# Splitting the MLP weights into fp16 halves: half of the scalings moved from ScalarE to GpSimd, and each subtraction in one instruction

## The reference

```python
scores = scale * np.matmul(q, k.transpose(0, 1, 3, 2))
kth = np.partition(scores, -top_k, axis=-1)[..., -top_k:-top_k + 1]
scores = np.where(scores >= kth, scores, -1000000000.0)
attn = softmax(scores);  x = attn @ v          # 2304 rows of 512
h = x @ w_in                                   # 512 x 2048
x = (np.maximum(h, 0.0) + alpha * np.minimum(h, 0.0)) @ w_out
```

## Time and profile before

| | us |
|---|---|
| median of 3 runs | 1148.4 |
| lowest and highest | 1143.76 and 1156.6 |
| the profiled execution, its own time | 1143.76 |
| its span, first to last instruction | 1142.0 |
| busy in the span: PE, DVE, ACT, POOL | 929.2, 913.3, 624.2, 430.4 |

### The profile page before, as it was taken

The page is one execution under the profiler, slowest core; times in us unless marked ns, Lnnn a source line. Parts: engine busy times, 40 slices in busy tenths (PEclk is TensorE's granted clock), DMA queues, the critical chain, the costliest instruction groups (busy, mean ns, idle before and its releaser), DMA issues.

```text
span 1142.0 us, 22616 instructions
## 1 busy us (share of the span) xinstructions
PE 929.2 (81%) x6288; PEld 621.1 (54%) x6289; DVE 913.3 (80%) x2061; ACT 624.2 (55%) x1291; POOL 430.4 (38%) x597
## 2 busy tenths in 40 slices
PE   5235578898899889888988898899888887499896
PEld 3123346575667557665766575666657565244343
DVE  4899979999999999999999999999999252311111
ACT  3775949637854784587469647845873461011010
POOL 0145637612841582167038514830681100101010
PEclk9666679999999999999999999999999899599899
DMA  7910201004001300310031013002000366444640
GB/s 210 354 32 3 50 22 33 22 2 118 7 21 53 73 0 21 92 34 21 1 102 23 21 34 91 0 21 73 23 1 1 116 222 226 139 162 142 219 145 18
DMA packets 98660, 84.08 MB, mean 74 GB/s; under 512 B 69116, under 2 KB 77308, under 8 KB 98048
## 3 DMA queue, kind: packets, MB, share of 16 engines
q1 hardware_dynamic: 94544, 78.56, 22.6%
q0 software_dynamic: 1488, 3.15, 0.8%
q10 hardware_dynamic: 2528, 1.18, 0.4%
HBM read 72.64 MB, written 11.53 MB: 74 GB/s over the span
## 4 chain that ended last, share of the span: by engine, by line
PE 57%; issue 10%; ACT 10%; POOL 10%; DVE 6%; DMA 4%; SPq 1%; POOLq 1%; ACTq 0%; DVEq 0%
PE acc L583 16%; PE acc L552 7%; PE sc L523 6%; PE acc L570 5%; PE pt_full L541 4%; POOL pos_part L347 4%; PE sc L687 3%; POOL arena L349 2%; PE pt_full L754 2%; ACT arena L821 2%; PE pt_full L762 2%; POOL arena L1317 2%; DMA arena<-in_moe_w_dram 2%; PE acc L592 2%; DVE best L1032 1%
## 5 line engine op out<-in xcount | busy, mean ns | idle before, releaser
L1032 DVE MAX8 best<-arena 128x8 f32<-128x576 f32 x576 | 403.5, 741 | 9.6 <-ACT arena L814 9.6
L1045 DVE MATCH_REPLACE8 arena<-best,arena 128x576 f32<-128x576 f32 x432 | 315.7, 738 | 0.0
L1317 POOL TENSOR_SCALAR arena<-arena,row_inv 128x576 f32<-128x576 f32 x144 | 106.1, 753 | 365.7 <-DVE row_inv L1065 365.7
L570 PE MATMUL acc<-arena 128*128 (+1 forms) x1536 | 202.5, 286 | 24.6 <-ACT neg_part L860 22.7
L583 PE MATMUL acc<-arena 128*128 128x288 f16 x1536 | 200.9, 288 | 2.9 <-DVE arena L351 2.9
L570 PEld LDWEIGHTS acc<-arena 128*128 128x128 f16 x1536 | 146.3, 98 | 75.5 <-issue 33.9
L583 PEld LDWEIGHTS acc<-arena 128*128 128x128 f16 x1536 | 148.9, 98 | 48.9 <-issue 9.7
L541 PE MATMUL pt_full<-ident,arena 128*128 128x128 f32 x576 | 99.7, 301 | 76.8 <-POOL arena L1317 36.1
L814 ACT ACTIVATE arena<-sc 128x576 f32<-128x576 f32 x144 | 92.1, 642 | 85.9 <-PE sc L523 69.5
L1053 DVE SCALAR_TENSOR_TENSOR arena<-arena,best 128x576 f32<-128x576 f32 x144 | 128.6, 940 | 6.4 <-ACT arena L821 6.4
L541 PEld LDWEIGHTS pt_full<-ident,arena 128*128 128x128 f32 x576 | 71.3, 152 | 106.7 <-issue 61.8
(11 more groups left out here) (170 smaller groups left out, 1025.1 us busy)
## 6 DMA issues: line engine op xcount, KB each, us to landing
arena<-in_moe_w_dram SPq DMA_DIRECT2D x64, 512.0 KB
nat<-in_v_dram SPq DMA_DIRECT2D x64, 128.0 KB, 2.2
nat<-in_k_dram SPq DMA_DIRECT2D x60, 128.0 KB, 2.8
x_rows<-x2n SPq DMA_DIRECT2D x24, 192.0 KB, 2.4
out_dram<-x2n SPq DMA_DIRECT2D x24, 192.0 KB, 2.6
nat<-in_q_dram SPq DMA_DIRECT2D x64, 64.0 KB, 2.1
arena<-in_moe_w_in_dram SPq DMA_DIRECT2D x4, 1024.0 KB, 7.4
arena<-in_moe_w_out_dram SPq DMA_DIRECT2D x4, 1024.0 KB, 13.3
```

The lines of the kernel that those rows point to most:

```text
L570: last = nc.tensor.matmul(dst[:, 0:HALF], win16[:, a, d, f * P:(f + 1) * P], xT16[:, bass.ds(row + d, 1), b, :].rearrange("p b s -> p (b s)"),
L1032: nc.vector.max(best[:, gp, j, r, :], src).then_inc(max_found if r == 0 else dve_step, 1)
L1045: nc.vector.match_replace(left[:, j, :], best[:, gp, j, r, :], src, MASKED).then_inc(dve_step, 1)
L1317: nc.gpsimd.tensor_scalar(probs[:, gp, j, :], probs[:, gp, j, :], row_inv[:, gp, j:j + 1], 1.0, ALU.mult, ALU.mult)\
```

## The change

POOL now scales the even splits (0, 2, 4, 6) itself, with a TENSOR_SCALAR of 128x2048 ahead of the subtraction (`scale_raw`). ACT waits for it (`w_scaled`), writes the high half, and then scales the odd split that follows (`w_scaled_too`). The high half of the odd split stays where it was, among the copies, and no scaling stands ahead of it there. Each low half is one subtraction of 128x2048 instead of four of 128x512.

```diff
--- before.py
+++ after.py
@@ -242,6 +242,7 @@
         folded = sem("folded")
         w_summed = sem("w_summed")
         v_summed = sem("v_summed")
+        w_scaled_too = sem("w_scaled_too")
         raw_loaded = [sem(f"raw_loaded{i}") for i in range(DT + OUT_CHUNKS)]
         maxima_ready = sem("maxima_ready")
         top_ready = sem("top_ready")
@@ -324,7 +325,6 @@
 
 
         SPLITS = DT + OUT_CHUNKS
-        SPLIT_PARTS = 4
         assert V_CHUNKS * P * STAGE == B * H * S * D and FT1 * DM == OUT_CHUNKS * F1 and V_CHUNKS % 2 == 0
         W_SLOT, V_SLOT = 0, 1
         split_slots = {n: [2 * n - 4, 2 * n - 3] for n in range(2, 6)}
@@ -903,14 +903,17 @@
 
             def high_weights(i, par, g, half):
                 for n in split_slots.get(GROUPS * (2 * i + par) + g, ())[half:half + 1] if isinstance(i, int) and i < MLP_LAG else ():
-                    k = 1 if n < DT else 2
-                    act.wait_ge(scale_ready, 1)
-                    act.wait_ge(raw_loaded[n], 16)
-                    nc.scalar.activation(raw[:, n, :], raw[:, n, :], ACT.Copy, scale=scale[:, k:k + 1]).then_inc(w_scaled, 1)
-                    act.wait_ge(w_scaled, n + 1)
+                    if half == 0:
+                        act.wait_ge(w_scaled, n // 2 + 1)
+                    else:
+                        act.wait_ge(w_scaled_too, n // 2 + 1)
                     if n:
                         act.wait_ge(w_ready, n)
                     nc.scalar.activation(split_target(n, 0), raw[:, n, :], ACT.Copy).then_inc(hi_ready, 1)
+                    if half == 0:
+                        k = 1 if n < DT else 2
+                        act.wait_ge(raw_loaded[n + 1], 16)
+                        nc.scalar.activation(raw[:, n + 1, :], raw[:, n + 1, :], ACT.Copy, scale=scale[:, k:k + 1]).then_inc(w_scaled_too, 1)
 
             def step(i, items, mlp, first=False, final=False):
 
@@ -1324,13 +1327,18 @@
                     nc.gpsimd.tensor_tensor(xT16[:, row, 1, :].rearrange("p b s -> p (b s)"), x32[:, c, :],
                                             xT16[:, row, 0, :].rearrange("p b s -> p (b s)"), ALU.subtract).then_inc(x_ready, 1)
 
+            def scale_raw(n):
+                k = 1 if n < DT else 2
+                pool.wait_ge(scale_ready, 1)
+                pool.wait_ge(raw_loaded[n], 16)
+                nc.gpsimd.tensor_scalar(raw[:, n, :], raw[:, n, :], scale[:, k:k + 1], 1.0, ALU.mult, ALU.mult).then_inc(w_scaled, 1)
+
             def split(n):
 
+                if n % 2 == 0:
+                    scale_raw(n)
                 pool.wait_ge(hi_ready, n + 1)
-                for part in range(SPLIT_PARTS):
-                    at = slice(part * F1 // SPLIT_PARTS, (part + 1) * F1 // SPLIT_PARTS)
-                    last = nc.gpsimd.tensor_tensor(split_target(n, 1)[:, at], raw[:, n, at], split_target(n, 0)[:, at], ALU.subtract)
-                last.then_inc(w_ready, 1)
+                nc.gpsimd.tensor_tensor(split_target(n, 1), raw[:, n, :], split_target(n, 0), ALU.subtract).then_inc(w_ready, 1)
 
             def share_maxima(lo, hi):
 
```

## The result

| | before | changed |
|---|---|---|
| median of 20 runs, us | 1148.39 | 1155.55 |
| lowest and highest | 1141.08, 1156.6 | 1150.42, 1161.04 |
| ratio of the changed kernel, 95% interval | | 1.0069 (1.0054 to 1.0086) |
| start of search 7 in the profiled execution | 161.44 | 169.13 |
| last `row_inv` | 887.17 | 894.69 |

The start of search 7 is the measure that I use throughout: the first MAX8 of search 7 on DVE, by then all the changed code is behind. It came 7.7 us later, and at the end of the searches DVE was 7.5 us late. That is the whole difference of the medians (7.2 us, 0.69% of 1148.4 is 7.9).

The account below looks back on a forecast made before the run. VectorE sets the loop's pace, with 6.1 us of slack before it; blocking by long POOL instructions uses that up and adds 10 us, giving 1153.8 from the profiled execution or 1158.4 from the median; forecast 1157, range 1147 to 1167.

Parts of the forecast that it names:

- rival A: POOL does not hold the shared port for a whole long instruction; only +1.6 us remains, 1150 us; chance 0.22.
- What bounds the kernel: VectorE paces the loop; before it, a late POOL/ACT chain makes VectorE wait 6.1 us for the exponentials of search 6.
- (1): ACT before the loop loses four of eight scalings, 4 x 1.99 us; the other four move behind a high half.
- (2): POOL gains four scalings of 128x2048, taken as 2.4 us each, between estimates of 2.1 and 2.7.
- Rival B: POOL's scaling runs no faster than its subtraction, 4.5 us for 2048: +17 us, 1165 us; chance 0.13.
- (3): On POOL, four subtractions of 512 become one of 2048, taken as 4.4 us instead of 4.49.
- (4): Walk through searches 2 to 6: long POOL instructions block VectorE, +10.9 us (8.4 to 12.7), less up to 1.5 own error.
- (5): ACT waits for POOL's scaling ahead of high halves 0, 2, 4, 6; alone, +1.6 us at the exponentials 6.
- With pieces of 1.12 us such a wait costs at most 1.1: VectorE multiplies, neg_max and row_den wait only until the running POOL piece ends, so at most 1.1 us.
- Rival C: Faster, as ACT loses 8 us and POOL piece overheads: 1142 us from the wait alone, at most 11.5 us gained; chance 0.05.

Follow-up runs that it names:

- norm_first: Kernel before, with normalise 5 between low halves 6 and 7 on POOL and PE's weights wait moved into the loop: 0.9954 of before.
- sub_four: Changed kernel with each subtraction in four pieces of 512 columns again, POOL's scaling left whole: 0.9998 of before, search 7 at 160.22.
- both_four: Changed kernel with subtraction and POOL's scaling both in four pieces of 512 columns: 1.0018 of before, search 7 at 161.97.
- all_pool_no_den: norm_first with all eight scalings on POOL in four pieces each and every row_den addition left out: 1.0045 of before.
- all_pool: all_pool_no_den with the row_den additions kept, POOL's pieces back to back: 1.0058 of before, search 7 at 166.86.
- all_pool_paused: all_pool_no_den with POOL waiting for its own last piece after every piece of 512 columns: 0.9985 of before, search 7 at 159.46.

## Why the prediction was right

The forecast was +10 us, in a range of +7 to +13 for that case; the medians moved by 7.2, search 7 by 7.7. The time lies in the range, and the class (within 1%) was the likeliest one. That the forecast of 1157 us came within 1.5 us of the median is in part luck: 1157 was picked between two sums (1153.8 and 1158.4) and is only 8.6 above the median of before, not 10. And the range, 1147 to 1167, takes in rival A's 1150 as well, so the time alone would not have told the two apart; the rows of the profile do. By its steps:

- What bounds the kernel: right. The wait of 6.1 us and its chain (low half 7, normalise 5, exponentials 6) were confirmed by norm_first, the loop's pace by its unchanged windows.
- (1), ACT's relief, is worth nothing: right. ACT then waited 6.69 us for `neg_max` of search 5.
- (2), the scaling: taken as 2.4, between 2.1 and 2.7; it measured 1.98, below the lower bound. The slope over the two smaller rows (0.9 ns an element) was the better guide, and the value should have been taken there. Rival B fell with it.
- (3), the subtraction: taken as 4.4, it measured 4.07. These two sizes are the term that was mis-sized. Put between the walk's own three results (10.9, 8.4 and 12.7), the measured sizes give about 8.0, an estimate; search 7 came 7.7 later. So the walk needed no further 1.5 us taken off; with the 1.5 off it gives 6.5.
- (4), the walk: every hold that it named came, at its place: scale product 3.91 (to 86.3 foretold, 85.29 seen), `neg_max` 3 1.53, `row_den` 4 3.75, a multiply of search 4 2.83, `row_den` 5 3.87, `neg_max` 5 1.52, a multiply of search 5 4.60. The starts of searches 3 to 6 were foretold as 87.1, 106.0, 128.5, 155.3 and came at 85.60, 103.84, 126.49, 152.25; search 7, 171 to 172, came at 169.13. Two thirds of the surplus are there by search 4, from the long durations; a walk in which each hold moves the next carries such an error to the end and doesn't average it.
- (5), the added wait of ACT, put at +1.6: sub_four and both_four, which keep it, start search 7 at 160.22 and 161.97 against 161.44. Neither is a difference that one profile shows.
- "With pieces of 1.12 us such a wait costs at most 1.1" was true of the kernel before and is not true in general, as all_pool_no_den shows.
- Rival A fell: the hold does last for the whole long instruction. The rule of the Trainium skill (SBUF — State Buffer, "Who interferes with whom") that the first to start holds the pair for its whole instruction agrees with the `row_den` of 3.75 us under a subtraction of 4.06. The holds of 13.24 and 13.32 us, each over fifteen POOL instructions, are more than this rule gives.
- Rival C: no gain came; where pieces were short (sub_four) the moved scaling was a draw.

That the chance of "slower by over 1%" was 0.29 was generous: it rested on the upper ends of both durations, which a look at the slope would have cut.

## What to carry to other kernels

When POOL and DVE work side by side, look for tiny DVE instructions with long durations before you look at waits: that is where the hold shows, and a merge that saves POOL 0.4 us can cost DVE 4. Work out first which of the two chains has slack, because the same hold is free in one kernel and whole in the next. And where POOL issues many instructions in a row beside a busy DVE, a wait on its own last one, 0.12 us each here, is worth a try: in the one kernel that has it, no hold outlasted one instruction.

## What the runs showed of the hardware that I had not expected

- A DVE multiply waiting beside a row of back to back POOL instructions of 0.68 and 1.12 us can be passed over again and again: 13.24 and 9.52 us in one kernel, 13.32 in another. In most places it gets in after one (1.70 us). What decides between the two was not found: three cases are too few, and the row_den additions are not it, since all_pool has them. With pauses of 0.12 us on POOL it never happened in one profiled execution.
- One POOL subtraction of 2048 columns takes 4.07 us where four of 512 take 4.50, and one scaling 1.98 where four take 2.70. The saving is real (0.4 and 0.7 us) and was worth less than nothing here.
- Reciprocals were never held, at 0.15 us beside a running subtraction, also where they took the place of a `row_den` that was held for 3.75.
- Which instructions are held follows neither from the name of the operation nor from its size alone. From the timeline of DVE in all_pool_paused, while a POOL subtraction runs from 82.52 to 84.07:

```profile
83.55 0.15 DVE L1097 TENSOR_SCALAR scale<-power 128x1 int32<-128x1 int32 x1
83.62 0.47 DVE L1112 TENSOR_TENSOR x_scale<-unscale 128x1 f32<-128x1 f32 x1
```

A TENSOR_SCALAR of 128x1 was not held, here or in the changed kernel (0.15 us at 81.31, under the subtraction of 81.22), while those of 128x3 (`row_den`, `neg_max`) were. Whether the width or the int32 type decides is not shown.
